# A second, small test on the eight largest candidates in each phase of a routed layer's search, and other steps for its row tiles and lists

## The reference

```python
def _attn_ref(q, k, v, i_gate, f_gate, o_gate):   # B, H, S, D = 4, 8, 768, 40: a gated linear recurrence
    ...
def _moe_ref(x, w_gate, w1, w2):                  # x 3072 x 320, 8 experts, hidden 1024
    cap = N // E
    logits = x @ w_gate
    order = np.argsort(-logits.flatten())
    for idx in order:
        tok, e = (int(idx) // E, int(idx) % E)
        if assigned[tok] >= 0 or counts[e] >= cap:
            continue
        assigned[tok] = e
        counts[e] += 1
    for e in range(E):
        mask = assigned == e
        out[mask] = np.maximum(x[mask] @ w1[e], 0.0) @ w2[e]
    ...
def _moe2_ref(x, w_gate, w1, w2):                 # each token to its largest logit, scaled by its probability
    ...
```

## Time and profile before

| | us |
|---|---|
| median of 3 runs | 941.03 |
| lowest, highest | 939.99, 944.13 |
| profiled execution | 942.81 |
| its span | 941.1 |
| TensorE busy | 764.7 |
| VectorE busy | 528.6 |
| GpSimd busy | 415.2 |
| ScalarE busy | 352.5 |

### The profile page before, as it was taken

The page is one execution under the profiler, slowest core; times in us unless marked ns, Lnnn a source line. Parts: engine busy times, 40 slices in busy tenths (PEclk is TensorE's granted clock), DMA queues, the critical chain, the costliest instruction groups (busy, mean ns, idle before and its releaser), DMA issues. The chain is left out here.

```text
span 941.1 us, 18647 instructions
## 1 busy us (share of the span) xinstructions
PE 764.7 (81%) x5612; PEld 708.6 (75%) x5612; DVE 528.6 (56%) x1627; ACT 352.5 (37%) x929; POOL 415.2 (44%) x558
## 2 busy tenths in 40 slices
PE   0599999996327896869779899925898988988997
PEld 0499999996216685758668889925898988988996
DVE  5277777775775555655565454213563646645643
ACT  3555555552013241413323444513342433433421
POOL 3277777774042552443525476651250513523511
PEclk9999999998557986988988999956999999999999
DMA  9955555540042421122222354354523245245110
GB/s 158 121 90 88 88 88 88 88 68 26 9 140 68 149 81 55 53 64 90 81 89 83 97 162 128 101 177 132 172 86 114 66 125 159 84 120 171 34 42 16
DMA packets 147691, 90.51 MB, mean 96 GB/s; under 512 B 112477, under 2 KB 138590, under 8 KB 147616
## 3 DMA queue, kind: packets, MB, share of 16 engines
q1 hardware_dynamic: 132560, 57.35, 27.8%
q10 hardware_dynamic: 10736, 19.61, 6.6%
q0 software_dynamic: 4320, 12.62, 4.1%
HBM read 74.31 MB, written 16.88 MB: 97 GB/s over the span
## 5 line engine op out<-in xcount | busy, mean ns | idle before, releaser
L600 ACT ACTIVATE l_hh<-bank 128x256 fp32r<-128x256 f32 (+1 forms) x200 | 83.2, 416 | 224.5 <-PE bank L585 223.6
L544 POOL TENSOR_TENSOR parts_w2l<-all_w,parts_w2h 128x320 fp32r<-128x320 f32 x128 | 120.2, 960 | 94.0 <-ACT parts_w2h L531 80.8
L604 DVE SCALAR_TENSOR_TENSOR l_hl<-bank,l_hh 128x256 fp32r<-128x256 f32 (+1 forms) x200 | 93.1, 467 | 112.3 <-ACT l_hh L600 110.3
L581 PE MATMUL bank<-l_xh,parts_w1h 128*128 128x256 f32 (+1 forms) x400 | 127.1, 318 | 20.5 <-DVE l_xh L574 15.5
L582 PE MATMUL bank<-l_xl,parts_w1h 128*128 128x256 f32 (+1 forms) x400 | 122.3, 306 | 0.0
L583 PE MATMUL bank<-l_xh,parts_w1l 128*128 128x256 f32 (+1 forms) x400 | 122.3, 306 | 0.0
L1418 POOL DMA_INDIRECT out<-l_y,l_ids x34 | 33.6, 987 | 167.4 <-DVE l_y L1494 162.4
L581 PEld LDWEIGHTS bank<-l_xh,parts_w1h 128*128 128x128 f32 x400 | 77.4, 194 | 26.7 <-DVE l_xh L574 13.4
L591 PE MATMUL bank<-parts_w2h,l_hh 128*128 128x320 f32 x272 | 87.1, 320 | 0.0
L538 POOL TENSOR_TENSOR parts_w1l<-all_w,parts_w1h 128x384 fp32r<-128x384 f32 x72 | 70.4, 1006 | 36.8 <-ACT parts_w1h L524 36.8
L592 PE MATMUL bank<-parts_w2l,l_hh 128*128 128x320 f32 x272 | 85.2, 313 | 0.0
(11 more groups left out here) (237 smaller groups left out, 1879.7 us busy)
## 6 DMA issues: line engine op xcount, KB each, us to landing
all_w<-in_moe_w SPq DMA_DIRECT2D x10, 1280.0 KB, 6.5
all_w<-in_moe_w SPq DMA_DIRECT2D x10, 1024.0 KB, 5.4
all_w<-in_moe_w ACTq DMA_DIRECT2D x6, 1280.0 KB, 11.8
all_w<-in_moe_w ACTq DMA_DIRECT2D x6, 1024.0 KB, 5.5
l_raw<-rows SPq DMA_DIRECT2D x18, 320.0 KB
all_w<-in_moe_w SPq DMA_DIRECT2D x20, 256.0 KB, 6.1
att_X<-in_o_gate SPq DMA_DIRECT2D x24, 160.0 KB, 4.0
att_q<-in_q SPq DMA_DIRECT2D x24, 160.0 KB, 3.2
```

Of the source, the lines that this page charges most:

```text
L544: ops.tensor_tensor(sh.w2l[:, r, p, :], sh.w2[:, p, :], sh.w2h[:, r, p, :].bitcast(FP), ALU.subtract).then_inc(sh.w2_low, 1)
L581: T.matmul(dst, sh.w1h[:, r, k, f], xh[:, k, :], start=k == 0, stop=False)
L600: return nc.scalar.activation(hh, src, ACT.Relu)
L604: return nc.vector.scalar_tensor_tensor(hl, src, 0.0, hh.bitcast(FP), ALU.max, ALU.subtract)
```

## The change

Each phase's first test has 64 pivots (128 in phase 0, which has two such tests one after the other, without the loop). Its bounds give new pivots of all 128 partitions; `few_pivots` puts them in a row, `compare_few` takes the eight largest with `V.max` and compares, `count_few`, `reached_few` and `codes_few` follow, and `bounds_few` asks the question. The loop stays for what is left then. The compares are three pieces of eight tiles. In a body `list_rows`, `sides`, `row_tile`, `route`, `ranks` and `places` stand at other steps, and GpSimd's `scatter` stands ahead of `low_w1`. Three operations with a value per partition as their scalar (`same`, `bits`, `hit`) become ones with two tensors.

```diff
             for e in range(NE):
-                low_w2(e, range(0, 5))
+                low_w2(e, range(0, 3))
                 if e + 1 < NE:
                     gather(e + 1)
-                low_w2(e, range(5, FT))
-                low_w1(e + 1, range(FT))
+                low_w2(e, range(3, FT))
                 if e:
                     scatter(e - 1)
+                low_w1(e + 1, range(FT))
...
+                more_rows = e + 1 < NE
                 for f in range(FT):
                     act.wait_ge(up_psum, FT * e + f + 1)
                     hidden_high(nc, hh[:, f, :], p_up[f % 2][:, 0:CAP]).then_inc(hh_done, 1)
+                    if f == 1 and more_rows:
+                        sides(e + 1)
                     high_w2(e, (f,))
                     if f in (2, 4, 6) and e:
                         result(e - 1, f // 2 - 1)
-                    if f == 2 and e + 1 < NE:
-                        sides(e + 1)
-                high_w1(e + 1, range(0, 3))
+                if more_rows:
+                    row_tile(e + 1, 0)
+                high_w1(e + 1, range(0, 2))
+                if more_rows:
+                    row_tile(e + 1, 1)
+                high_w1(e + 1, range(2, 4))
+                keep(e, 0)
+                if more_rows:
+                    row_tile(e + 1, 2)
+                high_w1(e + 1, range(4, 6))
                 if e:
                     exps(e - 1)
-                keep(e, 0)
-                if e + 1 < NE:
-                    row_tile(e + 1, 0)
-                high_w1(e + 1, range(3, 6))
-                if e + 1 < NE:
-                    row_tile(e + 1, 1)
                 keep(e, 1)
                 high_w1(e + 1, range(6, FT))
-                if e + 1 < NE:
-                    row_tile(e + 1, 2)
...
+            def bounds(width, row):
+
+                V.tensor_scalar(uc[:, 0:width], p_b[:, 0:width], 0.5, BIG, ALU.is_ge, ALU.mult)
+                V.tensor_scalar(lc[:, 0:width], p_b[:, 0:width], 0.5, -BIG, ALU.is_lt, ALU.mult)
+                d()
+                V.tensor_tensor_reduce(uc[:, 0:width], uc[:, 0:width], row, 1.0, upper[:, :], ALU.add, ALU.min, upper[:, :])
+                V.tensor_tensor_reduce(lc[:, 0:width], lc[:, 0:width], row, 1.0, lower[:, :], ALU.add, ALU.max, lower[:, :])
+                d()
+                V.tensor_scalar(dead[:, :], v[:, :], upper[:, :], -BIG, ALU.is_ge, ALU.mult)
+                V.tensor_tensor(hit[:, 0:width], lc[:, 0:width], lower[:, :].to_broadcast([P, width]), ALU.is_equal)
+                d()
+                V.tensor_tensor_reduce(dead[:, :], v[:, :], dead[:, :], 1.0, -4 * BIG, ALU.add, ALU.max, pivot[:, :])
...
+                bounds(width, p_a[:, 0:width])
+                dve.reg_add(rnd, rnd, 1)
+                d()
+                V.drain().then_inc(few_ready, 1)
+                codes(width)
+
+            def compare_few(k):
+
+                dve.wait_ge(few_psum, k + 1)
+                V.max(few[:, :], p_a[:, 0:P])
+                d()
+                V.tensor_tensor(above_few[:, :, :], few[:, :].unsqueeze(1).to_broadcast([P, NT, FEW]),
+                                v[:, :].unsqueeze(2).to_broadcast([P, NT, FEW]), ALU.is_le).then_inc(above_few_ready, 1)
+
+            def reached_few(k):
+
+                dve.wait_ge(cnt_few_psum, k + 1)
+                V.tensor_scalar(reach_few[:, :], p_b[0:NE, 0:FEW], float(CAP), None, ALU.is_ge).then_inc(reach_few_ready, 1)
+
+            def bounds_few(k):
+
+                dve.wait_ge(reach_few_psum, k + 1)
+                bounds(FEW, few[:, :])
+                question(FEW)
...
+                width = PIVOTS if k else P
+                if k == 0:
+                    for i in range(AC):
+                        compare(slice(i * NT // AC, (i + 1) * NT // AC), P)
+                    reached(P)
+                    dve.wait_ge(reach_psum, dve.snap(rnd) + 1)
+                    bounds(P, p_a[:, 0:P])
+                    dve.reg_add(rnd, rnd, 1)
+                    d()
+                    V.drain().then_inc(pivots_ready, 1)
+                    codes(P)
+                for i in range(3):
+                    compare(slice(i * LAST, (i + 1) * LAST), width)
+                reached(width)
                 if k:
                     list_rows(k - 1)
-                bounds()
+                first_bounds(k, width)
+                compare_few(k)
+                reached_few(k)
+                bounds_few(k)
                 decide()
...
+                k, more_rows = routes(e), e + 1 < NE
                 low_hidden(e, 0)
+                if more_rows:
+                    list_bases(e + 1)
                 low_hidden(e, 1)
-                if e + 1 < NE:
-                    list_bases(e + 1)
                 if k:
                     matches()
                 low_hidden(e, 2)
...
                     choices()
                 low_hidden(e, 3)
                 if k:
-                    compare(0)
+                    compare(slice(0, LAST), PIVOTS)
                 low_hidden(e, 4)
+                if more_rows:
+                    list_rows(e + 1)
+                low_hidden(e, 5)
                 if k:
-                    compare(1)
-                low_hidden(e, 5)
-                if e + 1 < NE:
-                    list_rows(e + 1)
-                if k:
-                    compare(2)
+                    compare(slice(LAST, 2 * LAST), PIVOTS)
                 low_hidden(e, 6)
                 if k:
-                    compare(3)
+                    compare(slice(2 * LAST, NT), PIVOTS)
                 low_hidden(e, 7)
                 if k:
-                    compare(4)
-                    compare(5)
+                    reached(PIVOTS)
+                if more_rows:
+                    row_tile(e + 1, 0)
+                if k:
+                    first_bounds(k, PIVOTS)
+                    compare_few(k)
+                if more_rows:
+                    row_tile(e + 1, 1)
+                if k:
+                    reached_few(k)
+                    bounds_few(k)
+                if more_rows:
+                    row_tile(e + 1, 2)
                 if e:
                     route(e - 1)
-                if k:
-                    reached()
-                    bounds()
-                if e + 1 < NE:
-                    row_tile(e + 1, 0)
                 if k:
                     decide()
                     more()
                     close(k)
-                if e + 1 < NE:
-                    row_tile(e + 1, 1)
+                if e:
+                    gates(e - 1)
+                    places(e - 1)
                 if k:
                     listed_tokens(k)
                     if k < NE - 2:
                         next_pivots()
                     else:
                         remaining(NE - 1)
-                if e + 1 < NE:
-                    row_tile(e + 1, 2)
-                if e:
-                    places(e - 1)
             route(NE - 1)
...
+            def few_pivots(k):
+                pe.wait_ge(few_ready, k + 1)
+                T.matmul(p_a[:, 0:P], pivot[:, :].to_broadcast([P, P]), ident[:, :], start=True, stop=True).then_inc(few_psum, 1)
+
+            def count_few(k):
+                pe.wait_ge(above_few_ready, k + 1)
+                for j in range(NT):
+                    mm = T.matmul(p_b[0:NE, 0:FEW], choice[:, :, j], above_few[:, j, :], start=j == 0, stop=j == NT - 1)
+                mm.then_inc(cnt_few_psum, 1)
+
+            def codes_few(k):
+                pe.wait_ge(reach_few_ready, k + 1)
+                T.matmul(p_b[:, 0:FEW], code_w[:, :], reach_few[:, :], start=True, stop=True).then_inc(reach_few_psum, 1)
 
...
+                    if f == 0 and more_rows:
+                        list_bases(e + 1)
+                    if f == 2 and more_rows:
+                        list_rows(e + 1)
+                    if f == 2 and k:
+                        pe.wait_ge(pivots_ready, k + 2)
+                        pivots(PIVOTS)
                     if f in (1, 3, 5) and e:
                         result(e - 1, f // 2)
-                    if f == 4 and e + 1 < NE:
-                        list_rows(e + 1)
-                    if f >= 5 and k:
-                        if f == 5:
-                            pe.wait_ge(choices_ready, k + 1)
-                        count(f - 5)
+                    if f == 5 and k:
+                        pe.wait_ge(choices_ready, k + 1)
+                        count(slice(0, LAST), PIVOTS)
+                    if f == 7 and k:
+                        count(slice(LAST, 2 * LAST), PIVOTS)
 
...
+                        at = j * FT + f
+                        if at == 0 and more_rows:
                             row_tile(e + 1, 0)
-                        if (j, f) == (1, 4) and k:
+                        if at == 0 and k:
+                            count(slice(2 * LAST, NT), PIVOTS)
+                        if at in (1, 3, 5) and e:
```

(24 more changed lines are left out.)

143 lines of the change are left out of this document (73 added, 70 removed).

## The result

The kernel before took 940.5 us in this comparison, the changed kernel 1037.8 us: a ratio of 1.101 [1.094, 1.109]. The profiled execution of the changed kernel took 1041.5 us with a span of 1039.8, against 941.1 before. The forecast of 976 had the sign and was 62 us short, and the time lies outside the range of 946 to 994. Experiments 3, 10 and 12 have one or two disturbed executions that are longer than their others, and what is said of these experiments rests on the others.

The account below looks back on a forecast made before the run. TensorE, busy 81% of the span, was taken to bound the kernel, with the search lengthening bodies. Terms by stretch, mainly waits from GpSimd's new order, summed to +35 us on 941.0: 976, range 946 to 994.

Parts of the forecast that it names:

- The rounds: Search loop: extra rounds stay in bodies 1 and 3, the one in body 2 goes, -10 us.
- GpSimd's order as the main term: low_w1 behind scatter on GpSimd: bodies 6 and 7 start 4 us later; VectorE held, +4.5 in bodies 5 and 6.
- Ahead of the bodies: Stretch before body 0: second test of phases 0 and 1, its bounds held by GpSimd's run, +6.5 us.
- A: Rival: the wait for low_w1 does not bind and the hold goes; about -26 us, 915; chance 0.14.
- B: Rival: VectorE's hold falls between GpSimd's subtractions and only the start waits; +18 us, 959; chance 0.12.
- C: Rival: the second test answers also in phases 3 and 5; -21 us, 955; chance 0.06.
- E: Rival: the edits cancel, within 0.5%; chance 0.04.
- Rival D: As forecast, and the waits let the clock fall in more of each body; +10 to +20 us, 990; chance 0.09.
- The forecast's own bounds: 963 and 987 us, said to be 5 us for the second test in five bodies and 4 for phase 1.
- the flag: Search's answer about 15.5 us after the down products' start: -0.5, +1.5, +3, +0.5 in bodies 1 to 4, +1.5 in body 0.
- row tile 0 at position 0: Down products: row tile 0 waits for its gather, +1.5 us in bodies 5 and 6, +0.5 elsewhere.
- the hold: GpSimd's subtractions hold VectorE's L1000 of list_bases: +4.5 us in bodies 5 and 6, +1.5, +3, +3 in 2 to 4.

Follow-up runs that it names:

- experiment 3: Changed kernel with 128 pivots in place of 64 in the first test of every phase: 1001.3 us, ratio 1.058.
- experiment 10: Changed kernel with products of constants filling TensorE's waits ahead of row tile 0 (bodies 5, 6) and at the start of bodies 5 to 7: 1030.2 us, ratio 1.089.
- experiment 12: Kernel before with the changed kernel's further tensors and semaphores allocated but unused: 945.4 us against 946.1, ratio 0.999.
- experiment 4: Changed kernel with the row tiles of bodies 5 and 6 at positions 4, 9 and 14 in place of 0, 4 and 9: 1023.9 us, ratio 1.085.
- experiment 9: Changed kernel with 34 products of constants filling TensorE's wait ahead of row tile 0 in bodies 5 and 6, every wait left: 1022.4 us, ratio 1.081.
- experiment 7: Changed kernel with GpSimd's order undone, 128 pivots, row tiles later in all bodies and no second test in phases 0 and 1: 923.9 us, ratio 0.978.

## Why the prediction was right in sign and wrong in size

**Right.** The rounds: the second test ends all phases but 3 and 5, so there are nine flags, with loops in bodies 1 and 3 alone. GpSimd's order as the main term: 55 us when undone, 47 us when done alone. The waits themselves: 4.1 and 3.8 us at the starts of bodies 6 and 7 for a forecast 4.0, 10.4 to 10.6 us from the last flag to the next start in bodies 1 to 4 for 11.0, and a hold to the run's end. Ahead of the bodies (+5.2 for +6.5) GpSimd's run held a step of the second test's bounds 6.29 us, and behind them (+5.3 for +5) it held L1067 of `route` 4.90 us, both as forecast. Body 7 (+1.6 for +1.5) is right for its reason too: 3.2 us of it are at 1.2 GHz behind a wait of 3.75. Rivals A, B, C and E are refuted: low_w1 binds, L1047 is held, the loops stay.

**Wrong: the clock.** The step that failed is that the sum took each wait at its own length, and left what runs behind it at the old clock, in every body but 7. Rival D, the clock, was put at 10 to 20 us in all and a chance of 0.09. Experiments 4 and 9 measured it in bodies 5 and 6: waits shorter by 2.3 us took 7.1 off a body, and with every wait left in place 4.4 to 6.1 came back. What the sum lacks in bodies 0 to 6 is 53 us, and they hold 108 us more at 1.2 GHz. For bodies 0 to 4 that rests on this arithmetic alone; no run filled a wait there. D was the right mechanism, 3 to 5 times too small if all of it is the clock's, and it was set up as an addition to the forecast though the forecast's own waits bring it about. The forecast's own bounds, 963 and 987, do not come out of the 5 and 4 us that they are said to be made of either, and nothing in them was the clock.

**Wrong: the flag, "about 15.5 us after the start of the down products in bodies 1 to 4".** It came 23.2, 23.3, 26.0 and 23.2 us behind it (body 2: 418.2 to 441.5). The positions between are paced by TensorE, and at 1.2 GHz three products of one take 0.80 us for 0.44: over 16 positions 5.8 us, and row tile 0's wait of 1.7 to 2.8 makes up the rest. With the order undone, 128 pivots and the tiles later (experiment 7) it is 17.6 to 17.9 in bodies 1 to 4. In body 0 the flag was forecast 1.5 us later in its body and came 6.7 later (33.4 us behind the body's start for 26.7), behind waits of 2.44 us at row tile 0, 1.61 at the second test's count and 1.50 at the question; the next start, 6.6 us behind the flag for a forecast 5.5, was sized right.

**Wrong: row tile 0 at position 0.** "+1.5 in bodies 5 and 6, +0.5 elsewhere": the wait measured 2.8 us in 5 and 6 and 1.7 to 2.8 in 0 to 4, where the kernel before, with this tile at position 9, had none over 0.25, and with its clock most of 7 us a body hung on it in 5 and 6 (experiment 4). Row tile 0 waits for all three transfers of the gather. In body 5 the third was issued at 17.6 us and landed at 20.7, much as the 3.1 of the earlier trace rows has it, but TensorE stood at the position at 17.9 and not at 19.4, since the hold ahead of it cost less than forecast. A tile was moved to just ahead of the landing of its rows.

**Wrong: the hold.** 4.5 us for bodies 5 and 6 was the time from one up group to the next, but TensorE's wait was 2.25, since it started late; taking the hold away gave 2.4 and 1.3 us. The forecast of +9 and +8 for these bodies thus held an error in the other direction, which hid part of the clock's. The reading of the earlier trace rows behind it was loose too: L1000 at 558.99 was 0.31 us ahead of the subtractions, but GpSimd was then at the last issue of its scatter (558.30 to 559.27), so the row does not show what an instruction does that starts with GpSimd idle. In bodies 2 and 4 the hold was under-sized, at 1.5 and 3, and put on the wrong instruction: the prediction moved `next_pivots` with the flag and did not ask what it would meet. Their up parts grew from 18.6 and 17.0 to 23.9 and 24.1 us.

**Wrong: "the second layer is not touched".** True of its lines; it was 11.6 us longer in the profiled execution. Cause open, see experiment 12.

## What to carry to other kernels

Price a new wait on TensorE as the wait and what runs behind it at half the clock: where a row of the kernel shows TensorE falling to 1.2 GHz behind a stop of that length, double the wait at least (2.8 us in experiment 4). A stop behind which the rows show the full clock costs itself (1.2 to 1.4 us here). A queue served in order (GpSimd's here) turns one swapped line into waits for the engine that feeds on it: before moving a transfer ahead of a computation ask what the transfer itself waits for. Count the positions from the landing of a gather and put its consumer behind them; where a wait can't go, it can be filled, unless another engine's wait follows at once.
